# Fused attention and two feed-forward blocks on one core: dense q, and local scores in 64x64 tiles

## The reference, cut to what matters

```python
q_d, k_d, v_d = (x.reshape(B, H, S // 4, 4, D).mean(axis=3) for x in (q, k, v))   # B 4, H 8, S 576, D 64
out_up = np.repeat(sm_attn(q_d, k_d, v_d), 4, axis=2)        # attention over 144 pooled tokens
mask = np.abs(pos[:, None] - pos[None, :]) < 4               # local attention: 3 keys to each side
scores = np.where(mask, scale * np.matmul(q, k.transpose(0, 1, 3, 2)), -1e9)
out_local = np.matmul(softmax(scores), v)
x = (out_up + out_local) as (B * S, H * D)
x = moe(x)     # rms norm, silu(x @ w_gate) * (x @ w_val) @ w_out, 512 -> 1536 -> 512
y = moe2(x)    # relu(x @ w_in) ** 2 @ w_out, 512 -> 2048 -> 512
```

## Time and profile before

| | us |
|---|---|
| timed runs (3) | 1101.17, 1101.16, 1098.11; median 1101.16 |
| span of the profiled execution, first to last instruction | 1096.2 |
| PE busy | 1003.8 (92%) |
| DVE busy | 491.1 (45%) |
| ACT busy | 370.4 (34%) |
| mean granted TensorE clock, share of full | 0.967 |

### The profile page before, as it was taken

One profiled execution on the slowest core, in us unless ns is written; L12 is line 12 of the kernel. 1 busy time (PEld: TensorE's weight loads), 2 busy tenths in 40 slices (PEclk: granted clock), 3 DMA queues, 4 the chain that ended last, 5 costly groups with the idle time before them and its releaser, 6 DMA issues.

```text
span 1096.2 us, 19820 instructions
## 1 busy us (share of the span) xinstructions
PE 1003.8 (92%) x7140; PEld 953.4 (87%) x7140; DVE 491.1 (45%) x1116; ACT 370.4 (34%) x1098; POOL 158.3 (14%) x169
## 2 busy tenths in 40 slices
PE   3557586699999999999999999999999999999998
PEld 2557485589999999999999999899999999999997
DVE  4467586946453535344443433333333333333332
ACT  3354454454312121222222245423233233332322
POOL 5142334258000000000000048200000000000000
PEclk9798888889999999999999999999999999999999
DMA  7673542035100000000000026100000000000000
GB/s 143 176 142 77 118 80 69 1 109 151 30 1 1 1 1 1 2 1 1 1 1 1 2 69 168 35 1 21 20 1 20 1 19 19 0 19 19 0 20 20
DMA packets 39848, 42.82 MB, mean 39 GB/s; under 512 B 21600, under 2 KB 25696, under 8 KB 39200
## 3 DMA queue, kind: packets, MB, share of 16 engines
q1 hardware_dynamic: 39776, 41.83, 15.6%
HBM read 37.10 MB, written 4.72 MB: 38 GB/s over the span
## 4 chain that ended last, share of the span: by engine, by line
PE 81%; DMA 7%; DVE 7%; SPq 2%; issue 2%; ACT 1%; DVEq 0%; ACTq 0%
PE bank L989 45%; PE bank L1069 18%; PE bank L1018 14%; DMA vwin<-v_dram 7%; PE bank L941 2%; DVE xT L632 1%; SPq L258 1%; PE bank L897 1%; DVE vd L647 1%; SPq L247 1%; DVE mxd L607 1%; DVE xT L674 1%; DVE mxl L607 0%; PE bank L873 0%; DVE wsplitA L680 0%
## 5 line engine op out<-in xcount | busy, mean ns | idle before, releaser
L989 PE MATMUL bank<-xs,wsplitB 128*128 128x288 f32 (+1 forms) x3324 | 451.0, 289 | 0.0
L989 PEld LDWEIGHTS bank<-xs,wsplitB 128*128 128x128 f32 x3324 | 439.3, 188 | 9.4
L1069 PE MATMUL bank<-wsplitB 128*128 128x512 f32 x702 | 178.5, 390 | 0.0
L831 DVE TENSOR_TENSOR prod<-sig 128x256 f32<-128x256 f32 x144 | 61.3, 426 | 192.7 <-ACT sig L555 192.5
L1018 PE MATMUL bank<-hb,wsplitB 128*128 128x288 f32 x960 | 141.9, 297 | 2.7 <-ACT hb L475 2.7
L1069 PEld LDWEIGHTS bank<-wsplitB 128*128 128x128 f32 x702 | 123.8, 188 | 19.0
L1018 PEld LDWEIGHTS bank<-hb,wsplitB 128*128 128x128 f32 x960 | 131.7, 188 | 4.2 <-POOL wsplitB L381 3.3
L475 ACT CAST hb<-prod 128x288 fp32r<-128x288 f32 x96 | 41.6, 433 | 255.9 <-DVE prod L780 255.9
L555 ACT ACTIVATE sig<-bank 128x256 f32<-128x256 f32 x144 | 55.3, 384 | 198.3 <-PE bank L989 198.2
L780 DVE TENSOR_TENSOR prod<-prod,bank 128x288 f32<-128x288 f32 x96 | 43.6, 454 | 174.1 <-PE bank L989 174.0
L941 PE MATMUL bank<-probT,vwin 70*128 70x128 f32 x288 | 45.2, 307 | 66.3 <-DMA vwin<-v_dram 51.1
(11 more groups left out here) (82 smaller groups left out, 850.2 us busy)
## 6 DMA issues: line engine op xcount, KB each, us to landing
wraw<-w_dram SPq DMA_DIRECT2D x62, 256.0 KB, 2.8
vquad<-v_dram SPq DMA_DIRECT2D x4, 1152.0 KB
out_dram<-work SPq DMA_DIRECT2D x18, 256.0 KB, 2.0
vwin<-v_dram SPq DMA_DIRECT2D x28, 140.0 KB
kp<-k_dram SPq DMA_DIRECT2D x8, 320.0 KB, 4.4
qz<-q_dram SPq DMA_DIRECT2D x32, 80.0 KB, 3.9
kp<-k_dram SPq DMA_DIRECT2D x8, 256.0 KB, 8.4
qz<-q_dram SPq DMA_DIRECT2D x32, 64.0 KB, 3.7
```

The source lines that it names most:

```text
L831: nc.vector.tensor_tensor(prod[:, tp, 0:C2], sig[:, tp, 0:C2], sig[:, tp, 0:C2], ALU.mult).then_inc(s_done, 1)
L989: last = mm(bank[:, 0:cols], wslot(n)[:, pw, 128 * k:128 * k + 128], x[:, px, k, 0:cols], start=(i == 0 and k == 0), stop=(i == 2 and k == ...
L1069: last = mm(OUT[par][tt][:, :], gs[:, px, 128 * tt:128 * tt + 128], w[:, pw, :], start=(m == 0 and i == 0), stop=(m == J2 - 1 and i == 2))
```

## The change

q is loaded dense into `qs` (a head on its 64 partitions, 576 tokens), by one DMA where four stood. The zero fills go. A local unit's scores are made by matmuls that use 64 rows and 64 columns of the array: for each half (even heads, odd heads) one mask matmul, and for each pair and half one score matmul with 64 queries stationary and 70 keys moving. The readers of q for the pooled sums (`sum_q` on GpSimd, `sum_last_q` on VectorE) take the dense layout. TensorE's loop over batches 1 and 2 is written out by Python in place of a loop on the engine.

```diff
-        qz = sb("qz", [128, NP, NL, 2, QB], stack=att)
+        qs = sb("qs", [128, NP, S], stack=att)
...
-                        for p in range(NP):
-                            sp.dma_start(qz[rows, p, t0 // QB:t1 // QB, h, :],
-                                         q_d[b, :, 2 * p + h, t0:t1].rearrange("d (u s) -> d u s", s=QB)
-                                         ).then_inc(q_in, 16)
+                        sp.dma_start(qs[rows, :, t0:t1], q_d[b, :, h::2, t0:t1]).then_inc(q_in, 16)
...
-                src = qz[rows, :, blocks, h, :].rearrange("p a u (s r) -> p a u s r", r=FACTOR)
+                src = qs[rows, :, tokens].rearrange("p a (u s r) -> p a u s r", s=QS, r=FACTOR)
...
-            for u0, u1 in ((0, SA_COLS // QB), (SA_COLS // QB, NL)):
-                nc.vector.memset(qz[64:128, :, u0:u1, 0, :], 0.0)
-                nc.vector.memset(qz[0:64, :, u0:u1, 1, :], 0.0).then_inc(zeroed, 1)
...
-                    mm(bank[:, :].rearrange("p (a b) -> p a b", a=NP)[:, :, 0:KW], identb[:, :],
-                       mask[:, which, :].rearrange("p (a b) -> p a b", a=NP), start=True, stop=False,
-                       skip_group_check=True)
+                    halves = [slice(64 * h, 64 * h + 64) for h in range(2)]
+                    for rows in halves:
+                        mm(bank[rows, :].rearrange("p (a b) -> p a b", a=NP)[:, :, 0:KW], identb[rows, rows],
+                           mask[rows, which, :].rearrange("p (a b) -> p a b", a=NP), start=True, stop=False,
+                           skip_group_check=True)
                     for p in range(NP):
-                        last = mm(bank[:, KC * p:KC * p + KC], qz[:, p, i].rearrange("p h s -> p (h s)"),
-                                  kp[:, p, QB * i:QB * i + KC], start=False, stop=True, skip_group_check=True)
+                        for rows in halves:
+                            last = mm(bank[rows, KC * p:KC * p + KW], qs[rows, p, QB * i:QB * i + QB],
+                                      kp[rows, p, QB * i:QB * i + KW], start=False, stop=True, skip_group_check=True)
...
-            with pe.Fori(1, B - 1) as b:
+            for b in range(1, B - 1):
                 batch(b, False)
```

More of the change, by code:

```diff
@@ L349, in sum_q @@
                 blocks = slice(u, NL) if part else slice(0, u)
+                tokens = slice(SA_COLS, S) if part else slice(0, SA_COLS)
                 dst = qd[rows, :, blocks, h, :]
-                src = qz[rows, :, blocks, h, :].rearrange("p a u (s r) -> p a u s r", r=FACTOR)
+                src = qs[rows, :, tokens].rearrange("p a (u s r) -> p a u s r", s=QS, r=FACTOR)
                 if n in (0, 6):
-                    pool.wait_ge(qb_in if part else qa_in, 32 * NP * (b + 1))
+                    pool.wait_ge(qb_in if part else qa_in, 32 * (b + 1))
                     if not b0:
@@ L649, in sum_last_q @@
             def sum_last_q(b, p, b0):
-                dve.wait_ge(qb_in, 32 * NP * (b + 1))
+                dve.wait_ge(qb_in, 32 * (b + 1))
                 if not b0:
@@ L655, in sum_last_q @@
                 blocks = slice(SA_COLS // QB, NL)
-                src = qz[64:128, p:p + 2, blocks, 1, :].rearrange("p a u (s r) -> p a u s r", r=FACTOR)
+                src = qs[64:128, p:p + 2, SA_COLS:S].rearrange("p a (u s r) -> p a u s r", s=QS, r=FACTOR)
                 nc.vector.reduce_sum(qd[64:128, p:p + 2, blocks, 1, :], src, AX).then_inc(kd_done, 1)
@@ L877, in qk @@
                 if i in (0, SA_COLS // QB):
-                    pe.wait_ge(qb_in if i else qa_in, 32 * NP * (b + 1))
-                    if b0:
-                        pe.wait_ge(zeroed, 2 if i else 1)
+                    pe.wait_ge(qb_in if i else qa_in, 32 * (b + 1))
                 if i in (0, SA_COLS // QB - 1):
@@ L904, in qk @@
                         if b0:
-                            pe.wait_ge(zeroed, 3)
+                            pe.wait_ge(zeroed, 1)
                     for a in range(NQ):
```

## The result

The changed kernel takes 1106.42 us (median of 5 runs, 1104.21 to 1111.86) against 1100.78 of the kernel before on the same chip (1098.11 to 1101.17): ratio 1.0070, 95% interval 1.0048 to 1.0091 (the two medians by themselves are 5.6 us or 0.5% apart). The forecast was 1095.7, faster. The profiled execution has a span of 1102.4 us and a time of its own of 1104.21, the lowest of the five; the mean granted TensorE clock of the five is 0.943 to 0.956, where the profile of before had 0.967.

What follows compares the result with a forecast made beforehand. The prediction took feed-forward matmuls for 77% of the span and, in attention, the waits for vwin's single DMA engine as the bound; -5.5 - 1.6 + 1.6 = -5.5 us gave 1095.7 us, range 1090.5 to 1101.5.

Steps and rivals of the forecast that it cites:

- The likeliest case: Whole kernel: faster by 5.5 us, to 1095.7 us (-0.5%); chance 0.5.
- twelve DMAs fewer at the start: Start, SP's queue: first vwin issues at 6.0 instead of 14.05 us and is ready earlier, -5.5 us.
- scores in 64x64 tiles: Local units: only unit 5, at half clock behind vwin's landing, gains: -0.4 us a batch, -1.6 over four.
- larger DMAs in the loop: Batch loop: more of the next batch's part 0 under way slows vwin, +1.6 us, taken between 0 and +3.7.
- the rest: Part 1 loads, pooled sums and TensorE's written-out loop: no effect, 0 us.
- What bounds attention: a single DMA engine behind vwin: Attention: vwin's 67-row windows go through one engine each; TensorE waits four times, 51.1 us in all.
- VectorE sets the pace from unit 6 on, only unit 5 counts: Local units: VectorE takes 2.63 us an iteration, TensorE 2.34; scores are on the path only at unit 5.
- my lower bound of 3.3: Start: smallest gain expected for the first vwin, 3.3 us, with k and q at 216 GB/s.
- Rival 3: After each vwin wait: clock stays low longer, +2.0 us a batch per further half-clock iteration, 8 over four; chance 0.1.

Runs made afterwards that it cites:

- split_before: The kernel before, TensorE's loop written out, with each 67-row window of vwin loaded by two DMAs of 64 and 3 rows: 1053.84 us, 0.9591.
- before_unrolled: The kernel before with TensorE's loop over batches 1 and 2 written out, nothing else: 1098.90 us, 0.9998 of the kernel before.
- tiles_only: The kernel before with its padded q and 20 DMAs a batch, but 64x64 score tiles and TensorE's loop written out: 1104.92 us, 1.0065.
- dense_only: The changed kernel with dense q and 8 DMAs a batch, but full-array score matmuls of 128 columns (output not the reference's): 1100.42 us, 1.0010.
- late_pad: The changed kernel with part 0 issued after vwin has landed and 120 instructions more at the start of TensorE's program: 0.9971 of the kernel before.

## Why the prediction was wrong

The likeliest case and its sign were wrong. The profiled spans set the terms side by side (us, of 1096.2 and 1102.4):

| term | forecast | in the two profiles |
|---|---|---|
| twelve DMAs fewer at the start | -5.5 | -0.5, at the end of batch 0 |
| scores in 64x64 tiles | -1.6 | +2.0, first to last values of batches 1 to 3 (-0.07, +1.55, +0.51), with the clock in it |
| larger DMAs in the loop | +1.6 | +2.2, last to first values (+0.8, +1.2, +0.2) |
| the rest | 0 | +2.5 behind attention: 1.2 in the stops and 1.5 in the stretch at lower clock, which kernels without the change have too; 0.2 came back later |

So two steps failed, the term at the start and the rest at nothing, and a third, the scores, was undone by the clock. Step by step:

- *What bounds attention: a single DMA engine behind vwin.* Right: split_before takes all but the first of the four waits away (4.3 us are left of that one) and is 45 us faster. *VectorE sets the pace from unit 6 on, only unit 5 counts*: nearly right. In the changed kernel VectorE waits 0.53 us for TensorE at unit 6 too, since the clock is still low there; the 0.29 us that a unit saves at full clock does not show, for batch 1 takes 24.16 us from first to last values against 24.23.
- *Twelve DMAs fewer at the start, -5.5*: the largest miss, 5.0 us of the 11.7 between forecast and profile. It has two parts. The landing came 2.8 us earlier, below my lower bound of 3.3: I had taken 339 and 216 GB/s for k and q, and behind 6 us the DMAs ran at 203 and 202. With 203 GB/s my own sum gives 2.6 (2.36 MB in 11.6 us, vwin ready at 12.4 for 14.95; an estimate from these rows). And of the 2.8 only 0.5 was left at the end of batch 0. wstage, last in SP's order, took 1.4, for its split had moved only from 47.17 to 45.75, and a stretch at half clock took 0.9. I had priced the wait that goes and not the next wait behind it.
- *Scores in 64x64 tiles, -1.6*: the price of the scores was better than forecast (1.31 us in place of 1.94 at half clock; from unit 5's mask to VectorE's start 1.43 us in place of 2.18, where I had 1.76), the more so as the halves share a PSUM bank and still overlap. The rule of the Trainium skill that I weighed (TensorEngine Tiling, Gotcha 1: PSUM Pressure) does not bind here: the two masks go to one bank, from different row tiles, in 0.44 us together, the time of one. But the gain did not arrive. In batch 1 the later return of the clock took it back within the next iteration, and batches 2 and 3 were longer than before.
- *Larger DMAs in the loop, +1.6*: right in mechanism and somewhat low: 0.9 and 1.2 us from first issue to values in batches 1 and 2. As foreseen, no DMA of part 0 sticks in SP any more; the four go out one behind the other while vwin is on its way:

```profile
75.68 0.60 SPq L245 DMA_DIRECT2D kp<-k_dram  x1
...
77.76 0.57 SPq L246 DMA_DIRECT2D qs<-q_dram  x1
```

- *The rest at nothing*: "TensorE's written-out loop drops register steps of its queue; it hides". I costed TensorE's longer program by what it executes and not by where it puts the code behind it. The loop is innocent (before_unrolled, 0.9998), but the tiles add 648 instructions (9 matmul records a unit more, each with a weight load, over 36 units), and where a loop jumps back 220 us later TensorE then stops twice. The stops cost 1.2 us in the changed kernel's profile; the ratio went from 1.0070 to 1.0021 with 120 instructions more, but not by the stops alone. No rival named it.
- *Rival 3, the clock stays low for longer*, had the sign and a part of the truth: batch 2 stayed at half clock for all of its local units. An iteration took 4.0 us there and not 4.7, and the batch lost 1.55 us in all and not 2 an iteration, for the iterations behind ran without the waits for VectorE's copies that the kernel before has there. At 0.1 it was too low. The forecast had the clock come back as soon as before; in the rows it stayed at 0.50 over 136 to 152 us with TensorE busy throughout.

tiles_only (1.0065) and dense_only (1.0010) show that the slowdown comes with the tiles. How its 0.70% divides between the clock in attention and the place of the code the runs leave open.

## What to carry to other kernels

A wait removed is worth what the next wait behind it leaves, so name that one with its time before booking the gain. Where a change adds instructions to an engine, look in the whole span for its idle time by "issue", above all where a loop jumps back, and try the kernel once with the code moved by some instructions before judging the change; then check that these did not shift anything else. Where the clock moves from one execution to the next, take more than one profile before giving a microsecond to a cause. And look at what the longest wait is made of before trimming the work beside it: two DMAs of 67 rows were worth 45 us, the whole redesign of the scores at best 3 (late_pad, 0.9971).

## What the runs showed of the hardware beyond this

- Idle for instructions: where a loop jumps back TensorE stopped for 0.8 to 2.8 us at a time, with a packet of the instruction queue some 3 us before it went on. Whether it stopped once or twice depended on 120 instructions at the start of the program.
- Leaving out 45% of the moving columns of full-array fp32 matmuls (128 to 70) saved 5% of their time (1.82 us for 1.91) and cost 1.4% of the kernel. The granted clock stayed at 0.50 through 24 us in which TensorE was busy for 19.5.
- Full-array idle work while waiting (140 or 90 matmuls) was worth 0.63%; it moves the later code too, and how much of the gain is the clock's isn't told apart.
- DMAs over 67 partitions trickled at 26 GB/s at a DMA share of 0.07; with 64 + 3 partitions the waits of the loop were gone. One engine for 67 is what the rule of the Trainium skill gives (DMA: Bandwidth & Descriptors, Why a DMA increments its semaphore by 16 and not by 1).
